# Three-stage attention and two-layer network on one core: where the slots without a layer-one product stand

## The reference

```python
q, k, v: (4, 8, 576, 64) float32, tau = 0.02
scores = q @ k.T / sqrt(64)
scores = where(scores >= max(scores) - tau, scores, -1e9)
attn = exp(scores - max(scores)); attn /= sum(attn) + 1e-9
x = (attn @ v) laid out as (2304 tokens, 512)
h = x @ w_in;  x = relu(h)**2 @ w_out           # layer one, w_in (512, 2048), w_out (2048, 512)
h = x @ w2_in; g = h * tanh(softplus(h)); out = g @ w2_out   # layer two, same sizes
```

## Time and profile before

| | |
|---|---|
| time, median of 3 runs (lowest to highest) | 1150.06 us (1149.76 to 1151.54) |
| the profiled execution: its time, its span | 1150.88 us, 1149.1 us |
| TensorE (PE) busy | 1105.6 us, 96% of the span |
| VectorE (DVE), ScalarE (ACT), GpSimd (POOL) busy | 66%, 56%, 51% |
| mean granted TensorE clock | 0.994 of full speed |
| DMA | 65.33 MB, mean 57 GB/s |

### The profile page before, as it was taken

How to read it: one execution, slowest core, us unless ns; L and a number is a source line. 1 busy time by engine, 2 the same in 40 slices (tenths; PEclk the granted TensorE clock), 3 DMA queues, 4 the chain that set the end, 5 groups by cost and what they waited for, 6 DMA issues and landing times.

```text
span 1149.1 us, 21018 instructions
## 1 busy us (share of the span) xinstructions
PE 1105.6 (96%) x7472; PEld 1040.9 (91%) x7472; DVE 759.2 (66%) x1977; ACT 645.4 (56%) x1230; POOL 586.2 (51%) x657
## 2 busy tenths in 40 slices
PE   5998899999999999999999999899999999999998
PEld 4776799999999999999999999889999999999997
DVE  5776677777677667676631014588787777878775
ACT  5786566665656566656543236555555555555554
POOL 5887788666766677676644445322222222222222
PEclk9999999999999999999999999999999999999999
DMA  5454322112222212121010204500101001010000
GB/s 147 130 153 113 92 74 72 53 49 70 55 71 58 60 47 81 44 69 53 20 50 11 92 2 146 156 19 1 56 1 56 1 1 56 1 55 1 28 1 28
DMA packets 73545, 65.33 MB, mean 57 GB/s; under 512 B 26080, under 2 KB 58848, under 8 KB 73440
## 3 DMA queue, kind: packets, MB, share of 16 engines
q1 hardware_dynamic: 68528, 58.98, 17.9%
q10 hardware_dynamic: 4912, 5.01, 1.3%
HBM read 49.81 MB, written 14.16 MB: 56 GB/s over the span
## 4 chain that ended last, share of the span: by engine, by line
PE 86%; DVE 4%; ACT 4%; issue 2%; DMA 2%; POOL 1%; SPq 0%; POOLq 0%; ACTq 0%; DVEq 0%
PE acc L130 8%; PE acc L131 8%; PE acc L132 8%; PE hidden L130 7%; PE hidden L132 7%; PE hidden L131 7%; PE pT L935 6%; PE scores L130 3%; PE scores L132 3%; PE scores L131 3%; PE pT L130 3%; PE pT L132 3%; PE pT L131 3%; PE outs L964 3%; PE outs L965 3%; PE scores L924 3%
## 5 line engine op out<-in xcount | busy, mean ns | idle before, releaser
L531 POOL TENSOR_TENSOR g_lo<-g,g_hi 128x384 fp32r<-128x384 f32 x96 | 97.9, 1020 | 314.0 <-ACT g_hi L562 314.0
L505 POOL TENSOR_SCALAR probs<-probs,inv_sum,flat 128x576 f32<-128x576 f32 x144 | 120.6, 839 | 130.8 <-DVE inv_sum L781 130.5
L130 PE MATMUL hidden<-x_hi,w_hi 128*128 128x256 f32 x576 | 170.6, 296 | 2.3 <-DVE x_lo L806 1.6
L130 PE MATMUL acc<-g_hi,w_hi 128*128 128x256 f32 x576 | 163.9, 285 | 0.2 <-POOL g_lo L526 0.2
L131 PE MATMUL acc<-g_lo,w_hi 128*128 128x256 f32 x576 | 162.9, 283 | 0.0
L132 PE MATMUL acc<-g_hi,w_lo 128*128 128x256 f32 x576 | 162.8, 283 | 0.0
L132 PE MATMUL hidden<-x_hi,w_lo 128*128 128x256 f32 x576 | 162.7, 282 | 0.0
L131 PE MATMUL hidden<-x_lo,w_hi 128*128 128x256 f32 x576 | 162.5, 282 | 0.0
L745 DVE TENSOR_SCALAR_CACHE_REDUCE s_neg<-scores 128x576 f32<-128x576 f32 x126 | 95.0, 754 | 71.5 <-PE scores L925 71.3
L521 POOL TENSOR_TENSOR rg<-rg 128x256 f32<-128x256 f32 x144 | 98.4, 683 | 75.4 <-ACT rg L636 74.5
L562 ACT ACTIVATE pt_hi<-pT 128x640 fp32r<-128x640 f32 x108 | 76.3, 707 | 71.0 <-PE pT L935 67.4
(11 more groups left out here) (116 smaller groups left out, 3106.5 us busy)
## 6 DMA issues: line engine op xcount, KB each, us to landing
k_raw<-kT SPq DMA_DIRECT2D x64, 144.0 KB, 2.9
q_raw<-qT SPq DMA_DIRECT2D x62, 144.0 KB, 3.0
y<-w_in SPq DMA_DIRECT2D x26, 256.0 KB, 2.8
y<-w_out SPq DMA_DIRECT2D x26, 256.0 KB, 3.1
x_raw<-x SPq DMA_DIRECT2D x36, 128.0 KB, 2.1
x<-y ACTq DMA_DIRECT2D x9, 512.0 KB, 2.9
x_raw<-x SPq DMA_DIRECT2D x6, 768.0 KB, 5.1
out<-y SPq DMA_DIRECT2D x18, 256.0 KB, 2.4
```

Source lines behind the costliest of these rows:

```text
L130: pe.matmul(out, a_hi, b_hi, start=first, stop=False, **flags)
L505: pool.tensor_scalar(probs[:, t, :], probs[:, t, :], inv_sum[:, t:t + 1], flat[:, t:t + 1], ALU.mult, ALU.add).then_inc(probs_ready, 1)
L531: pool.tensor_tensor(g2_lo[:, k % GRING, :], g2[:, k % 2, :], g2_hi[:, k % GRING, :].bitcast(F32), ALU.subtract).then_inc(g2_split, 1)
```

## The change

```diff
-BEGIN = [40, 58, 76, 94, 112, 130, 147, 163, 179]
+BEGIN = [40, 58, 76, 94, 112, 130, 148, 164, 180]
 BESIDE = 6
-STEP_AT = {BEGIN[b] + f + (f // 8 if b < BESIDE else 0): (b, f) for b in range(NB1) for f in range(FT)}
+STEP_AT = {BEGIN[b] + f + ((f + 1) // 8 if b < BESIDE else 0): (b, f) for b in range(NB1) for f in range(FT)}
...
-        READ_AT = {BEGIN[b + 1] + (0 if b + 1 < BESIDE else 1): b for b in range(NB1 - 1)}
+        READ_AT = {BEGIN[b + 1] + 1: b for b in range(NB1 - 1)}
```

## The result

The changed kernel takes 1164.03 us (median of 4 runs, 1163.58 to 1165.6), the kernel before 1149.91 (4 runs, 1149.23 to 1151.54): ratio 1.0119, 95% interval 1.0104 to 1.0133, so 12 to 15 us slower. Forecast were 1159.9, between 1154.0 and 1165.0. The direction and the place were right; the size was 9.85 us where 14.1 were measured by the medians.

What follows compares the result with a forecast made beforehand. TensorE, busy 96% of the span, was taken to bound the kernel, so the change acts only through waits. 8.07 + 0.97 + 0.81 = 9.85 us more gave 1159.9 us, range 1154.0 to 1165.0.

Steps and rivals of the forecast that it cites:

- What goes: Old light slots such as 84 and 86 become full; 0.66 us lost in each of 11 periods goes, 7.3 us.
- What comes: In the new light slots the weighing waits for the low part of its own slot; net sum 8.07 us more.
- slots 56, 74, ...: Light slots without first product, x_lo ahead of the row minimum; low part 3.64 after the transposes' start, 1.32 us lost each.
- slots 58, 76, ...: Light slots without second product; low part ends 2.86 us after the transposes' start, 0.49 us lost each.
- slots 67, 85, ...: Light slots without second product; low part ends 2.75 us after the transposes' start, 0.38 us lost each.
- slots 65, 83, 101, 119, 137: Light slots without first product; low part ends 2.81 us after the transposes' start, 0.49 us lost each.
- among the rivals with a chance of 0.12: GpSimd goes first at the mask in light slots without first product, holding it 0.8 us more; chance 0.12.
- Its smaller form: That rival in six slots of 0.8, 4.8 us more, 1164.7; the larger form took all twelve, 9.6, 1169.5.
- The first rival: Splitting x does not delay slots 56, 74, ...: 3.64 falls to 2.81, 4.15 us less, 1155.8; chance 0.16.
- The seam: Between blocks 5 and 6, slot 148's first product waits for x_lo, 0.97 us, and the next for the rectifying, 0.81.
- The second term: At the seam, slot 149's first product waits for the rectifying on the one `hidden` buffer, 0.81 us.
- Costed at nothing: Sums read a slot later, under 2.5 us of cover; five reads of 0.69 would cost 3.5 us without it.

Runs made afterwards that it cites:

- begin_only: The kernel before with the changed `BEGIN` and `READ_AT`, the steps inside blocks 0 to 5 as before; ratio 1.0011 to the kernel before.
- low_first_after: The changed kernel with VectorE's low part ahead of the mask instead of behind it; ratio 0.9949 to the kernel before.
- x_earlier: The changed kernel with the third part of the next block's x split one slot earlier; ratio 1.0118 to the kernel before.
- mask_first_x: The changed kernel, GpSimd's split of even heads' values held until the mask is done, third part of x split one slot earlier; ratio 1.0042 to the kernel before.
- steps_no_seam: The changed kernel with block 5 and the begin of block 6 as in the kernel before; ratio 1.0094 to the kernel before.

## Why the prediction was right, and where it fell short

**What goes** held: slots 84 and 86 became full and wait for nothing; by the slot lengths 7.5 us went, 7.3 were predicted. begin_only, which keeps those light slots, keeps their waits too.

**What comes** held in its mechanism: the weighing waits for the low part of its own slot. That the wait goes when the low part comes early (low_first_after) shows it rather than argues it. By its terms, loss of a slot against 3.68 (5.12 - 1.44) or 3.72 (5.16 - 1.44):
- slots 56, 74, ...: 1.32 predicted, 5.01 - 3.68 = 1.33 measured (1.31 in two of the five).
- slot 47: 1.06 predicted, 4.71 - 3.68 = 1.03.
- slots 58, 76, ...: 0.49 predicted, 4.19 - 3.72 = 0.47.
- slots 67, 85, ...: 0.38 predicted, 4.17 - 3.72 = 0.45; slot 49 lasts 4.32, which is 0.60.
- slots 65, 83, 101, 119, 137: **0.49 predicted, 4.88 - 3.68 = 1.20 measured. This is the step that was mis-sized**, "2.81 + 0.10 - 2.49 + 0.07". The 2.81 was read off a slot in which the mask won against GpSimd; in the changed kernel it lost in all five, and the low part ended at 320.33 - 316.80 = 3.53. Five times 0.71 are 3.6 us, more than the 2.9 by which the profiled executions exceed the forecast, and most of the 4.1 by the medians.

That this could happen stood among the rivals with a chance of 0.12. Its smaller form, 1164.7, comes near the measured 1164.03, in part by luck: it counted six slots of 0.8, and the runs show five of 0.71 (in slot 47, the sixth, the mask was held already before, and its 3.38 has that in it). So the time lies in the range, but the sum of the forecast left this cost out, and the range reached 1165.0 only because that rival's smaller form was taken into it. The argument against it was that all the timing ahead of it is tied to matmuls that stay. VectorE's is: the mask starts 0.88 after the transposes of its slot in every kernel with the mask in its old place. GpSimd's split of the values is not tied as closely: it starts 0.93 after them in the kernel before and 0.91 in the changed kernel and in begin_only, which has the old light slots. So the 2.81 was no property of the slot but one outcome of a race, and a held mask should have been counted as an equal case.

The first rival (x does not delay the slots) fell: 1.33 was paid in all five. But x alone was not the cause either, as x_earlier and mask_first_x show: behind it stood the mask.

**The seam** was 0.97 + 0.81 + 0.49 for slot 146, 2.27 in all. Measured by the distance of the late matmul from the one before, less the usual 0.12: 0.97, 0.63 and 0.43, 2.03. The rest of the trace grew by 1.7; the wait on `y` at the start of layer two is 0.6 shorter (4.8 for 5.4), and a wait of 0.3 on `g_lo` is new. The second term was too large: 0.81 predicted for the rectifying, 0.63 measured.

**Costed at nothing**: reading the sums a slot later, confirmed by begin_only. Not costed was a gain of 0.4 at slot 141, behind which the transposes had waited, because x_lo of block 6 stood ahead of the row minimum.

By the sum: stage 8.07 - 0.49 (slot 146) = 7.6 predicted, plus 3.6 for the mask, less the 0.4, is 10.8, and 10.6 was measured.

## What to carry to other kernels

When work is moved to shorten a short slot, look at which wait stands inside the slot that becomes short: a wait that a full slot hides (here the consumer at the end waits for a producer started at the beginning) comes into the open. Move the producer first (the low part ahead of the mask moved two lines and took 19 us of stage from the changed kernel, in which it had gone wrong; against the kernel before, the two edits together are worth 0.5%), then place the free slots; the two placements changed places in rank once that was done. And when a stretch read from one trace was decided by a race of some hundredths of a microsecond, put both outcomes into the sum.

## What the runs showed of the hardware

VectorE's mask (two SBUF inputs) against GpSimd's splits and squares: the mask takes 0.80 to 0.82 alone and from 0.9 up to 1.8 when held, by how much of a GpSimd operation it meets, while the low part (one input in PSUM) took 0.80 to 0.83 in all 108 slots of every kernel. By the rule of the Trainium skill named in the prediction (SBUF — State Buffer, Who interferes with whom) one side blocks the other, and the order of issue decides which. The traces agree that they exclude each other, nearly: in slot 83 of the kernel before, mask and split of the values together last from 313.28 to 314.84, 1.56 us, where 0.82 and 0.88 in a row are 1.70.

The starts of the records can't be that order: in the changed kernel the mask's record begins first, and the mask loses. But for this pair (the values' split right behind the queries', the mask right behind the row minimum) the distance of the two starts, which the traces hold to the nanosecond, goes with the outcome. The mask won where it was 0.045 us ahead (five slots, all in the kernel before) and lost where it was 0.028 to 0.035 ahead (25 slots, in the changed kernel, steps_no_seam, begin_only and x_earlier). The 358.42 and 358.46 of x_earlier are 0.035 apart, the 313.28 and 313.32 of the earlier trace rows 0.045. Between the two traces GpSimd's work ahead differs by about 0.01: its scaling of the rows in slot 82 took 0.834 in the kernel before and 0.822 in begin_only, with the same program in slots 82 and 83. What makes that difference, and whether the kernel before would fall the other way in another execution, stays open: each kernel has one trace.
